# Working each 128-token chunk of a linear-attention stage as two halves of 64, on 64x64 matmul tiles

## What is computed

```python
for t in range(S):                      # S = 768, D = 48
    kt, vt, rt = k[:, :, t], v[:, :, t], r[:, :, t]
    cur = einsum('bhd,bhe->bhde', u[None] * kt, vt)          # the bonus u of the token itself
    y[:, :, t] = einsum('bhd,bhde->bhe', rt, state + cur)
    state = w[None, :, :, None] * state + einsum('bhd,bhe->bhde', kt, vt)
```

## Time and profile before

| | us |
|---|---|
| three runs | 408.25, 412.22, 410.69 (median 410.69) |
| the profiled execution | 407.5, its span 405.7, mean granted clock 0.986 |
| first scores (L329) begin | 10.76 |
| scores of step 4 (chunk 1) begin | 32.39 |
| scores of the last step begin | 129.59 |

### The profile page before, as it was taken

The page is one execution under the profiler, slowest core; times in us unless marked ns, Lnnn a source line. Parts: engine busy times, 40 slices in busy tenths (PEclk is TensorE's granted clock), DMA queues, the critical chain, the costliest instruction groups (busy, mean ns, idle before and its releaser), DMA issues.

```text
span 405.7 us, 9085 instructions
## 1 busy us (share of the span) xinstructions
PE 388.6 (96%) x3234; PEld 308.7 (76%) x3234; DVE 236.0 (58%) x399; ACT 188.1 (46%) x432; POOL 119.0 (29%) x113
## 2 busy tenths in 40 slices
PE   5769999999999899999999999999999999999996
PEld 5658788878787654467888888888888888888885
DVE  6658867786867440028665655565656565555551
ACT  1034444444443313257656454645554464546452
POOL 5879887777756121014530000000000000000000
PEclk9589999999999999999999999999999999999999
DMA  7699999999999968990000100200020020002002
GB/s 238 240 391 335 347 337 313 316 322 316 328 313 344 372 226 297 405 376 10 2 0 27 53 0 2 78 0 0 0 78 0 0 78 0 0 0 78 2 0 78
DMA packets 28613, 63.89 MB, mean 158 GB/s; under 512 B 2640, under 2 KB 16576, under 8 KB 28208
## 3 DMA queue, kind: packets, MB, share of 16 engines
q1 hardware_dynamic: 27600, 63.12, 44.1%
q10 hardware_dynamic: 992, 0.49, 0.6%
HBM read 58.88 MB, written 4.72 MB: 157 GB/s over the span
## 4 chain that ended last, share of the span: by engine, by line
PE 64%; DVE 2%; issue 1%; ACT 1%; DVEq 0%
PE bank L569 16%; PE bank L571 16%; PE bank L570 16%; PE bank L556 5%; PE bank L495 3%; PE bank L476 3%; PE bank L316 1%; DVE glo L798 1%; PE bank L537 1%; PE bank L360 1%; DVE gf L792 1%; PE bank L486 0%; PE bank L440 0%; PE bank L504 0%; PE bank L381 0%
## 5 line engine op out<-in xcount | busy, mean ns | idle before, releaser
L792 DVE TENSOR_TENSOR gf<-bank,sg 128x512 f32<-128x512 f32 x96 | 66.2, 690 | 86.4 <-ACT sg L943 86.0
L569 PE MATMUL bank<-glo,whi 128*128 128x512 f32 x288 | 112.4, 390 | 0.2 <-DVE glo L798 0.2
L571 PE MATMUL bank<-ghi,wlo 128*128 128x512 f32 x288 | 112.1, 389 | 0.0
L570 PE MATMUL bank<-ghi,whi 128*128 128x512 f32 x288 | 112.1, 389 | 0.0
L943 ACT ACTIVATE sg<-bank 128x512 f32<-128x512 f32 x96 | 57.3, 597 | 94.0 <-PE bank L556 93.9
L798 DVE TENSOR_TENSOR glo<-gf,ghi 128x512 fp32r<-128x512 f32 x96 | 69.2, 721 | 0.2
L569 PEld LDWEIGHTS bank<-glo,whi 128*128 128x128 f32 x288 | 54.1, 188 | 12.3 <-DVE glo L798 1.1
L571 PEld LDWEIGHTS bank<-ghi,wlo 128*128 128x128 f32 x288 | 54.1, 188 | 11.3
L570 PEld LDWEIGHTS bank<-ghi,whi 128*128 128x128 f32 x288 | 54.1, 188 | 11.2
L949 ACT ACTIVATE ghi<-gf 128x512 fp32r<-128x512 f32 x96 | 59.9, 624 | 0.9 <-DVE gf L792 0.9
L835 ACT ACTIVATE yt<-bank 112x512 f32<-112x512 f32 x24 | 14.3, 598 | 68.9 <-PE bank L360 68.9
(11 more groups left out here) (121 smaller groups left out, 393.3 us busy)
## 6 DMA issues: line engine op xcount, KB each, us to landing
ring<-w SPq DMA_DIRECT2D x24, 512.0 KB, 5.9
rkb<-rk SPq DMA_DIRECT2D x23, 512.0 KB, 5.2
krb<-kr SPq DMA_DIRECT2D x24, 384.0 KB, 5.3
ring<-w SPq DMA_DIRECT2D x4, 1536.0 KB, 13.6
ring<-w SPq DMA_DIRECT2D x8, 768.0 KB, 9.7
vb<-v SPq DMA_DIRECT2D x24, 192.0 KB, 5.2
out<-ob SPq DMA_DIRECT2D x18, 256.0 KB, 2.1
ring<-win SPq DMA_DIRECT2D x3, 1024.0 KB, 14.0
```

Of the source, the lines that this page charges most:

```text
L569: pe.matmul(o, w_hi, lo, start=(f == 0), stop=False)
L570: pe.matmul(o, w_hi, hi, start=False, stop=False)
L571: pe.matmul(o, w_lo, hi, start=False, stop=(f == KF - 1)).then_inc(prod_ps, 1)
L792: dve.tensor_tensor(gf[:, f % 2, :], bank[f % 4][:, :], sg[:, f % 2, :], ALU.mult).then_inc(gf_ok, 1)
```

## The change

Each chunk is worked as two halves of 64 tokens with a state between them (`mid`). Scores are wanted within a half only, so the masks are half as large; every small product becomes one of at most 64 rows and 64 columns on one of the array's four 64x64 tiles. The bonus sums become products with a single moving column (`ucol`). r by token is no longer loaded, and neither is u spread over the partitions.

```diff
@@ loads @@
-                sp.dma_start(krb[:, b % 2, :, :, :], kr_v[n]).then_inc(kr_in[b % 2], 16)
-                wait(sp, st_ps, n - 3)
+                sp.dma_start(krb[:, b % 2, :, :], kr_v[n][:, 0, :, :]).then_inc(kr_in[b % 2], 16)
+                wait(sp, yt_ps, n - 3)
@@ hardware loop: two passes of eight steps instead of four passes of four @@
-            with eng.Fori(1, C - 1) as c:
-                for b in range(B):
-                    step(c, b)
+            with eng.Fori(0, (C - 2) // 2) as two:
+                for odd in (1, 2):
+                    for b in range(B):
+                        step(2 * two + odd, odd % 2, b)
@@ TensorE @@
-        SC, YT, ST, YN, LG = bank[0:4], bank[4], bank[5], bank[6], bank[7]
+        SC, YT, ST, YN, LG = bank[0:2], bank[2:4], bank[4:6], bank[6], bank[7]
+            def scores(c, par, b):
+                wait(pe, masked, 2 * n)
+                wait(pe, dd_ok, 2 * n)
+                pe.wait_ge(rks_ok, n + 1)
+                pe.sem_inc(tile_go, 1)
+                for hp in range(HP):
+                    for s in range(2):
+                        t = slice(SUB * s, SUB * s + SUB)
+                        for g in range(2):
+                            d = slice(64 * g, 64 * g + D)
+                            last = pe.matmul(SC[g][t, hp * SUB:(hp + 1) * SUB], rks[d, b % 2, 1, hp, t],
+                                             rks[d, b % 2, 0, hp, t], start=True, stop=True)
...
+            def bonus_sums(c, par, b):
+                pe.wait_ge(rkp_ok, n + 1)
+                pe.sem_inc(tile_go, 1)
+                # hp, s, g as above: 32 products of one column
+                            last = pe.matmul(SC[g][t, HP * SUB + hp:HP * SUB + hp + 1], rkp[d, b % 2, hp, t],
+                                             ucol[d, hp:hp + 1], start=True, stop=True)
...
+            def outputs(c, par, b):
+                # 32 products with st (first half) or mid (second half), 9 transposes of vd,
+                # 32 products of at and vb; waits and a tile_go ahead of each of the three
+                pe.wait_ge(rs_used, n + 1)      # ahead of the last 32: its own state products
...
+            def state(c, par, b):
+                # 32 products of kk and vb, 48 moving columns, one per head and half
...
+            def step(c, par, b):
+                scores(*here)
+                bonus_sums(*here)
+                if is_first(c, b):
+                    state(*here)
+                else:
+                    outputs(*prev(*here))
+                if not (is_last(c) and b == B - 1):
+                    state(*following(*here))
+                # turns, gather, tokens as before
@@ VectorE: the order of a step @@
+                scale(*here)
+                new_states(*here)        # mid = decayed st + ST[0]
+                # slot_max / running as before
+                bonus_copies(*here)      # two copies of 4 columns out of PSUM into dds
+                if not is_last(c):
+                    end_state(*here)     # st[next] = mid + ST[1]
+                mask(*here)              # of this step, two instructions of 256 columns
@@ ScalarE @@
-                act.activation(yt[0:PAIR, b, :, :].rearrange("p h t -> p (h t)"), YT[0:PAIR, :], ACT.Copy)\
-                   .then_inc(yt_ok, 1)
+                for p0, w, s, q0, x in ((0, PAIR, 0, 0, 0), (0, 64, 1, 64, 0), (64, 64, 1, 0, 1)):
+                    act.activation(yt[p0:p0 + w, b, :, SUB * s:SUB * s + SUB],
+                                   YT[s][q0:q0 + w, SUB * x:SUB * (x + HP)].rearrange("p (x t) -> p x t", x=HP),
+                                   ACT.Copy).then_inc(yt_ok, 1)
@@ GpSimd: one product of 112x512 by channel in place of two of 128x384 by token @@
+                pool.tensor_tensor(rkp[0:PAIR, b % 2, :, :], rkb[0:PAIR, b % 2, 0, :, :],
+                                   rkb[0:PAIR, b % 2, 1, :, :], ALU.mult).then_inc(rkp_ok, 1)
```

More of the change, by code:

```diff
@@ L374, in state, with tokens @@
                 last.then_inc(st_ps, 1)
-            def tokens(c, b):
+            def tokens(c, par, b):
                 n = B * c + b
-                wait(pe, yt_ok, n + 1)
+                wait(pe, yt_ok, 3 * n + 3)
                 wait(pe, yn_ok, 2 * n)
-                for hp in range(HP):
-                    last = pe.transpose(YN[:, hp * PAIR:(hp + 1) * PAIR], yt[0:PAIR, b, hp, :],
+                for x in range(HP):
+                    last = pe.transpose(YN[:, x * PAIR:(x + 1) * PAIR], yt[0:PAIR, b, x, :],
@@ L442, in spread_weights @@
                 last.then_inc(ct_ps, 1)
-            outputs(C - 1, B - 1)
-            tokens(C - 1, B - 2)
+            outputs(*last_of, B - 1)
+            tokens(*last_of, B - 2)
             pe.wait_ge(c_ok, 1)
@@ L448, in _ @@
             logits(C - 1)
-            tokens(C - 1, B - 1)
+            tokens(*last_of, B - 1)
             keep_warm(bank[3], 4)
@@ L729, in _ @@
             steps(dve, step)
-            mask(C - 1, B - 1)
             slot_max(C - 1)
@@ L817, in _ @@
             act.dma_start(idt[:, :], ident).then_inc(s_ident, 16)
-            for dst, src in ((keep[:, :], strict),
-                             (ubc[:, :, :].rearrange("p h e -> p (h e)"), u.partition_broadcast(P))):
-                act.dma_start(dst, src).then_inc(s_const, 16)
+            for s in range(2):
+                t = slice(SUB * s, SUB * s + SUB)
+                act.dma_start(keep[t, :], strict[t, t]).then_inc(s_const, 16)
+            with nc.allow_non_contiguous_dma(reason="384 numbers, once"):
+                for g in range(2):
+                    act.dma_start(ucol[64 * g:64 * g + D, :],
+                                  u.rearrange("(h g d) -> g d h", g=2, d=D)[g]).then_inc(s_const, 16)
             act.dma_start(phs[0:PAIR, :, :], phi).then_inc(s_phi, 16)
@@ L871, in row_exp, with step @@
                 act.activation(x, x, ACT.Exp).then_inc(cexp_ok, 1)
-            def step(c, b):
+            def step(c, par, b):
                 tail = not is_first(c)
+                here = c, par, b
+                if tail and b == 1:
+                    logit_copy(c - 1)
+                if not (is_last(c) and b == B - 1):
+                    decay(*following(*here))
                 if tail and b == 1:
@@ L879, in step @@
                 if not is_first(c, b):
-                    columns(*prev(c, b))
-                    if not is_last(prev(c, b)[0]):
-                        decay(*prev(c, b))
+                    columns(*prev(*here))
                     if tail and b == 1:
                         turned(c - 1)
-                    if not is_first(*prev(c, b)):
-                        rows(*prev(*prev(c, b)))
+                    if not is_first(*prev(*here)[::2]):
+                        rows(*prev(*prev(*here)))
             def high_weights(which, t):
```

338 lines of the change are left out of this document (181 added, 157 removed).

## The result

| | before | after |
|---|---|---|
| median of four runs, us | 410.37 (408.25 to 412.22) | 469.90 (467.47 to 476.18) |
| span of the profiled execution, us | 405.7 | 466.7 |
| mean granted clock | 0.986 | 0.850 |

What follows compares the result with a forecast made beforehand. TensorE was taken to bound the attention stage, transfers close behind. 407.5 - 11.2 + 0.5 + 1 + 0.3 = 398.1 us, or 401.3 against the median; 400 was predicted, with an 8 in 10 range of 389 to 418.

Steps and rivals of the forecast that it cites:

- What bounds the kernel now: Attention stage before the change: bound by TensorE, transfers close behind; a plain step takes 4.58 us without a hole.
- What a small product costs: TensorE's 64x64 tiles: four run beside each other, a round costs 58 ns, 14.5 ns a product.
- Rival 1: TensorE takes product and load at no less than 22.5 ns; plain step 4.93 us, total 415.7; chance 0.24.
- rival 2: Tiles do not run two by two (29 ns), or each wait drains the array; 425 to 436 us; chance 0.12.
- TensorE, part by part: TensorE's work in a plain step after the change: 3.65 us, against 4.58 before.
- The ring: Scores, bonus sums, copies, end state, masks and scale between TensorE and VectorE: sets a plain step at 4.17 us.
- 19 steps x (5.12 - 4.53): Attention stage, chunk extras included: each step falls from 5.12 to 4.53 us, 11.2 us saved.
- GpSimd: One product of 512 columns for two of 384: 1.38 us against 2.1, so GpSimd's work gets shorter.
- Transfers: A step moves 1.44 MB for 1.64; 4.17 us at 346 GB/s, a share of 0.92 of a 4.53 us step.
- rival 3: Transfers bind: shorter packets at 300 GB/s make a step 4.8 us; 403 to 406 us; chance 0.10.
- Start, loop and end: Outside the steady steps: start +0.5 us, one jump back in the eight-step loop +1 (0 to 5.3), end 0.3.
- Rival 4: Code loading: larger program stalls TensorE about 5.3 us once or twice; 402 to 409 us; chance 0.08.

Runs made afterwards that it cites:

- e13: Kernel before with one more wait a step, token transposes held until VectorE made the next step's bonus sums; 422.36 us, ratio 1.035.
- e5: Kernel after with a loop body of four steps instead of eight, the state's copy on ScalarE; 431.95 us, ratio 1.056.
- e8: Kernel before with 120 small fp32 products more at each step, in its loop; 632.96 us, ratio 1.547.
- e9: Kernel before with 120 small fp32 products more at each step, all 24 steps written out; 603.84 us, ratio 1.476.
- e4: Kernel after with the expert weights (512 KB a step) loaded only after the 24 steps; 469.84 us in a single run.
- e7: Kernel after, loop of eight steps, with bonus sums as four products of two columns instead of 32 instructions; 466.56 us, ratio 1.138.
- e10: Kernel before with 60 small fp32 products more at each step, in its loop; 480.22 us, ratio 1.178.
- e14: Kernel before with 30 small fp32 products (60 instructions) more at each step, no added wait; 428.44 us, ratio 1.043.
- e2: Kernel before with all 24 steps written out, no hardware loop; 409.47 us, ratio 1.003.
- e3: Kernel after with all 24 steps written out, no jump back; 465.86 us, ratio 1.137.
- e6: e5 with the bonus sums as four products of 112x128 and two columns, 8 matmul instructions for 32; 431.25 us, ratio 1.053.
- e12: e5 with one more wait a step, the next state product held until VectorE scaled the step after it; 455.26 us, ratio 1.111.
- e1: Kernel after with a loop body of four steps instead of eight, end state copied back by VectorE; 433.18 us, ratio 1.058.

## Why the prediction was wrong

*What bounds the kernel now*: right; the kernel before stands as read, and a wait put on TensorE there lengthens the plain step (5.44 us in e13 for 4.58).

*What a small product costs*: right. Groups of 32 at full clock took 0.44 to 0.60 us where nothing held them, which is 14 to 19 ns a start for 14.5 forecast (the 0.71 for `at` in e5's step above is longer; five other kept steps have 0.48 or 0.49); four tiles do run two by two. Rival 1 (22.5 ns at least) falls with the 8 ns of e8 as well, and so does rival 2 (groups of 0.93).

*TensorE, part by part*: 3.65 us a plain step was forecast, 3.86 measured in e5. *The ring*: forecast at 4.17, so that it would bind; it did not, in the step shown. Its instructions were shorter than priced (scale 1.21 to 1.30 for 1.36, masks 0.67 for 0.80 as a pair, copies 0.23 for 0.28) and lie some 0.07 over each other. With a chunk at 18.7 for the forecast 18.1, the step "19 steps x (5.12 - 4.53)" was about three quarters right, in code that is kept. *GpSimd* was mis-sized (2.08 for 1.38 us, beside VectorE's scaling) and left off the path: in e5's kept stretch it is busy for 43.37 of 53 us and waits 7.0 on `krb`, and TensorE's sums wait for its `rkp` eight times. That this is what the 18.7 has above the forecast 18.1 is likely, and not tested. *Transfers*: rival 3 falls; the share was 0.59, and 0.85 in e5.

**The step that failed is "Start, loop and end": "One jump back: +1, from 0 to a landing of 5.3."** I had counted 173 pairs a step, had the 14 packets of before and the limit of what is kept, and priced only the one jump. The jump itself came at the top of its range (two holes there, 3.08 and 2.10 us), and 24.9 us of holes stand elsewhere. What the body not being kept means is that every instruction is fetched: 346 a step, 1.35 packets. At a step of 4.5 us a packet would be due every 3.3 us, the very least that e9 shows between two of them, while the kernel after got one every 4.6 us (14 from 67 to 131 us). Each shortfall is a hole, 30.1 us in the stretch, and the rest of the loss is the clock. By the rate of e5's kept chunks 19 steps would be 19 x 18.7 / 4 = 89 us; measured are 150.0; less the holes some 31 us remain, which the half clock can account for (it was granted for about 105 of the 150 us). The two seem to feed each other: a slow step leaves more time for fetching, and the 7.9 us a step would be where they meet. That would fit e4 and e7, where neither fewer bytes nor fewer instructions moved it much; it is argued and not shown. Rival 4 had the kind right, "code loading", but its price of "a landing once or twice" was out by a factor of six to eleven, and no case had the clock in it. The range ended at 418.

On the page cited: the Trainium skill (Runtime: NRT & Kernel Launch, Instruction fetch mechanics) was right that a body of eight such steps is not held. Its room for 2048 instructions is not borne out: e10's body of about 1,640 was fetched at every second pass, while 1,160 (e14) and about 1,450 (e5) were kept. By it, crossing from one 16 KiB block to the next is mostly hidden. e2 agrees (409.47 us); the kernel after and e3 do not, with holes of up to 3.8 us. The measurement decides. The overhead for each matmul in the Trainium skill (TensorEngine Tiling (Array Packing), Instruction Overhead), taken as serial cost an estimate of 25 ns, is contradicted by 8 ns in e8.

**What stays open.** Why TensorE's clock stays at half while the rows show it busy without a hole (e6, 50 to 65 us; e10, 7 us of its kept stretch) isn't settled. That holes bring it down in the kernel of small tiles is shown (e12); whether the smallness has a part in it, and how long a hole it takes, is not. Nor is it settled why e10's body was kept at every second pass. No run that keeps the new arithmetic and has all its code kept from the first chunk was made: with a loop over all six chunks the first would still be fetched (e5's took 27.6 us from the first scores to the fifth, before 21.6), and kept chunks win 1.7 us each: by an estimate from these numbers 6.0 us lost and five times 1.7 won, some 2 us in all, half a per cent. No version here beats the kernel before.

## What to carry to other kernels

Count instructions, not only array time: matmuls and weight loads of one loop body, fp32 ones twice. If the body isn't kept, divide them by 256 and ask whether a packet every 3.3 us at best, 4.6 here, feeds the step; 144 in 5 us were free, 346 in 4.5 were not. Splitting products into small tiles gains array time and pays in instructions, and here the starved TensorE lost its clock as well, so that the loss was double the holes (61 us for 30); the number of packets on the queue of instructions and the idle time marked "issue" are the two lines to look at first.

## What the runs showed that was not expected

- The same kernel with its loop body halved (e1, e5) is 35 us faster with more instructions in each step: what is kept is worth more than a copy of 0.36 us a step on ScalarE.
- The same copy on VectorE took up to 2.28 us while GpSimd made its product, and GpSimd's product of 512 columns took 2.3 us beside VectorE's scaling but 1.26 and 1.27 in two of e5's steps. There the scaling ran beside `vd` instead, which then took 1.8 us for 0.83: whichever of the two runs beside the scaling is a us longer.
- In the kernel before with 120 small products, the loop (e8) was 29 us slower than the same written out (e9), though code was fetched in both: at this size a jump back to code that is not kept does cost, while the kernel after and e3 differ by 4 us, within their intervals.
- Waits that left TensorE idle for 5.9 us of 70 (e13) and 60 small instructions at every step (e14) each left the clock at 1.00 for those 70 us, while holes of mostly 1.2 to 1.7 us in e12 brought it to 0.67 to 0.91.
- Every hole of the kernel after ends 1.3 to 1.6 us (2.0 at the jump back) after a packet of instructions has landed, so it can be told from a wait on data by the packets alone.
